# Six lines moved in the order lists of an attention and expert kernel on one Trainium2 core

## The reference, cut to what matters

```python
B, H, S, D = 2, 8, 576, 64
scores = D ** -0.5 * q @ k.T                  # per batch and head, 576 x 576
kth = the 32nd largest score of each row
scores = where(scores >= kth, scores, -1e9)   # top 32 of 576
attn = exp(scores - max); attn /= attn.sum() + 1e-9
x = (attn @ v) as 1152 x 512
x = silu(x @ w_in) @ w_out                    # 512 -> 2048 -> 512
P = exp(x @ w_gate - max), then 8 rounds of row and column normalisation
out = sum over 8 experts of P[:, e] * (relu(x @ w1[e]) @ w2[e])   # 512 -> 1024 -> 512
```

## Time and profile before

| | |
|---|---|
| median of three runs | 1304.44 us |
| profiled execution | 1304.42 us, its span 1302.6 |
| TensorE busy | 1265.2 us (97%) |
| VectorE busy | 653.2 us (50%) |
| ScalarE busy | 458.6 us (35%) |
| GpSimd busy | 365.7 us (28%) |
| chain that ended last | TensorE 79%, VectorE 16% |

### The profile page before, as it was taken

How to read it: one execution, slowest core, us unless ns; L and a number is a source line. 1 busy time by engine, 2 the same in 40 slices (tenths; PEclk the granted TensorE clock), 3 DMA queues, 4 the chain that set the end, 5 groups by cost and what they waited for, 6 DMA issues and landing times.

```text
span 1302.6 us, 21366 instructions
## 1 busy us (share of the span) xinstructions
PE 1265.2 (97%) x8109; PEld 1119.5 (86%) x8109; DVE 653.2 (50%) x1557; ACT 458.6 (35%) x960; POOL 365.7 (28%) x319
## 2 busy tenths in 40 slices
PE   6999999999999999999999999999999999999999
PEld 5777787887887998899899899898898898998997
DVE  5999999999998237322222222222222222222222
ACT  4776666766766233022022032031131130220210
POOL 2774434524434223033032031131131130230300
PEclk9999999999999999999999999999999999999999
DMA  4875664654544643021021120020120220210001
GB/s 129 275 245 181 255 221 127 231 186 171 208 178 156 259 162 98 1 65 50 17 65 33 32 64 32 32 64 17 48 64 1 64 64 0 64 60 5 0 0 72
DMA packets 72929, 130.14 MB, mean 100 GB/s; under 512 B 42016, under 2 KB 42016, under 8 KB 63648
## 3 DMA queue, kind: packets, MB, share of 16 engines
q1 hardware_dynamic: 72864, 129.27, 29.3%
HBM read 110.12 MB, written 19.14 MB: 99 GB/s over the span
## 4 chain that ended last, share of the span: by engine, by line
PE 79%; DVE 16%; ACT 1%; SPq 1%; DMA 1%; issue 1%; POOL 1%; ACTq 0%; DVEq 0%
PE banks L409 25%; PE banks L411 24%; PE banks L410 24%; DVE stats L862 7%; DVE rest L873 6%; PE banks L477 2%; PE banks L444 1%; PE banks L453 1%; DVE g_f L927 1%; PE banks L470 1%; DMA q_nat<-in_q_dram 1%; SPq L333 1%; PE banks L500 0%; ACT pT L705 0%; PE banks L425 0%
## 5 line engine op out<-in xcount | busy, mean ns | idle before, releaser
L822 ACT ACTIVATE h_hi<-banks 128x384 fp32r<-128x384 f32 x192 | 94.4, 492 | 624.7 <-PE banks L411 624.7
L409 PE MATMUL banks<-x_lo,wu_hi 128*128 128x384 f32 x768 | 257.2, 335 | 0.0
L411 PE MATMUL banks<-x_hi,wu_hi 128*128 128x384 f32 x768 | 256.8, 334 | 0.0
L410 PE MATMUL banks<-x_hi,wu_lo 128*128 128x384 f32 x768 | 256.8, 334 | 0.0
L988 DVE SCALAR_TENSOR_TENSOR h_lo<-banks,h_hi 128x384 fp32r<-128x384 f32 x192 | 106.8, 557 | 281.7 <-ACT h_hi L822 281.7
L1087 POOL TENSOR_TENSOR wu_lo<-wu_raw,wu_hi 128x512 fp32r<-128x512 f32 x76 | 95.9, 1299 | 526.1 <-ACT wu_hi L761 519.1
L1030 DVE SCALAR_TENSOR_TENSOR y_acc<-banks,plan_e,y_acc 128x512 f32<-128x512 f32 x135 | 101.3, 751 | 272.3 <-PE banks L411 272.3
L409 PE MATMUL banks<-wd_lo,h_hi 128*128 128x512 f32 x576 | 227.9, 396 | 0.0
L411 PE MATMUL banks<-wd_hi,h_hi 128*128 128x512 f32 x576 | 227.8, 396 | 0.0
L410 PE MATMUL banks<-wd_hi,h_lo 128*128 128x512 f32 x576 | 227.8, 396 | 0.0
L862 DVE MAX8 stats<-rest 128x8 f32<-128x576 f32 x216 | 156.1, 750 | 0.7
(11 more groups left out here) (103 smaller groups left out, 1804.7 us busy)
## 6 DMA issues: line engine op xcount, KB each, us to landing
wu_raw<-in_moe_w_dram SPq DMA_DIRECT2D x32, 512.0 KB, 3.7
wd_raw<-in_moe_w_dram SPq DMA_DIRECT2D x32, 512.0 KB, 3.7
wu_hi<-kept_up_hi SPq DMA_DIRECT2D x14, 1024.0 KB, 5.6
wu_lo<-kept_up_lo SPq DMA_DIRECT2D x14, 1024.0 KB, 8.0
wd_hi<-kept_down_hi SPq DMA_DIRECT2D x14, 1024.0 KB, 6.3
wd_lo<-kept_down_lo SPq DMA_DIRECT2D x14, 1024.0 KB, 8.4
q_nat<-in_q_dram SPq DMA_DIRECT2D x64, 72.0 KB, 2.3
wu_raw<-in_moe_w_in_dram SPq DMA_DIRECT2D x8, 512.0 KB, 5.3
```

Of the source, the lines that this page charges most:

```text
L409: pe.matmul(to, a_hi, b_lo, start=first, stop=False)
L410: pe.matmul(to, a_lo, b_hi, start=False, stop=False)
L411: return pe.matmul(to, a_hi, b_hi, start=False, stop=last)
L822: act.activation(h_hi[:, f, CH * c:CH * (c + 1)], ps_up[:, at % UBANKS, 0:CH], ACT.Relu).then_inc(h_hi_done, 1)
```

## The change

It moves lines in the lists of all five queues and touches no instruction itself.

- SP: the load of the first half of the next unit goes out at the step behind the one that begins a unit (it was two behind), the second half and the keeping two behind (three). Half 0 of the last "down" unit of the first expert thereby falls into the loop, half 1 stays behind it.
- TensorE: the weighing of tile s-3 stands ahead of the scores of tile s+1.
- ScalarE: `copy_scores(s+1)` stands behind `exp_scores(s-2)`, a high part of g and `copy_output(s-3)`.
- GpSimd: the low pieces stand behind the low parts of the outputs and of g, and they are those of ScalarE's same step, not of the step before.

```diff
 # SP
+                if split_at(step - 1):
+                    stream, n = split_at(step - 1)
+                    load_split(stream, n + 1, 0)
                 if split_at(step - 2):
                     stream, n = split_at(step - 2)
-                    load_split(stream, n + 1, 0)
-                if split_at(step - 3):
-                    stream, n = split_at(step - 3)
                     load_split(stream, n + 1, 1)
                     if n < SLOTS:
                         keep_unit(stream, n)
...
-            for half in range(2):
-                load_split("down", UQ + 1, half)
+            load_split("down", UQ + 1, 1)
 # TensorE
+                if 0 <= step - 3 < ALL:
+                    weigh_values(step - 3)
                 if step + 1 < ALL:
                     scores_of(step + 1)
-                if 0 <= step - 3 < ALL:
-                    weigh_values(step - 3)
 # ScalarE
                 take_slice(slice_at(step, 0))
-                if step + 1 < ALL:
-                    copy_scores(step + 1)
                 if 0 <= step - 2 < ALL:
                     exp_scores(step - 2)
                 g_high(slice_at(step - 1, 1))
                 if 0 <= step - 3 < ALL:
                     copy_output(step - 3)
+                if step + 1 < ALL:
+                    copy_scores(step + 1)
                 split_pieces(pieces_at(step, 0))
 # GpSimd
                     lower_scores(step - 2)
-                if step <= ALL:
-                    split_pieces(pieces_at(step - 1, 0))
-                    split_pieces(pieces_at(step - 1, 1))
                 if step % NT == 3 and NT <= step < ALL + NT:
                     output_lows(step // NT - 1, 2)
                 g_low(slice_at(step - 1, 0))
                 g_low(slice_at(step - 1, 1))
+                if step < ALL:
+                    split_pieces(pieces_at(step, 0))
+                    split_pieces(pieces_at(step, 1))
```

## The result

The changed kernel took 1319.2 us (median of 5 runs, 1318.45 to 1321.45), the kernel before 1306.11 on the same chip (5 runs, 1304.42 to 1306.95). The ratio is 1.0107, 95% interval 1.0093 to 1.012: slower, as forecast, with the forecast time of 1318.8 us met to 0.4 us. The profiled execution of the changed kernel took 1318.84 us, its span is 1317.0; before it was 1302.6, so that 14.4 us are to be found in the trace.

What follows compares the result with a forecast made beforehand. VectorE's searches, later with TensorE, were taken to set the attention stage's pace, TensorE alone the expert stage's. 1304.4 + 11.0 (GpSimd's low pieces) + 3.4 (TensorE's order) + 0 gave 1318.8 us, range 1307 to 1323.

Steps and rivals of the forecast that it cites:

- The ring: GpSimd and ScalarE wait in turn, steps 2 to 16: rounds of 6.00 us against VectorE's 5.28, 11.0 us lost.
- Its high bound: Upper bound of the ring's cost, with more time for output copies and a later copy_scores in seven steps: 13.7 us.
- VectorE's wait in the ring: VectorE would wait for copy_scores (L862) or an exponential (L888), some 0.8 us a step from about step 5 on.
- TensorE's order: Weighing first makes TensorE wait for ScalarE's copy: 0.68 us in five rest-tile steps without a first slice, 3.4 us.
- The five others without a slice: There TensorE later waits 1.06 us for VectorE's slice, which takes up the 0.68 us: cost 0.
- ScalarE's order: Exponential ahead of copy_scores on ScalarE: could return the 0.3 us wait at L888, taken as 0.
- SP's order: Earlier weight loads could mend only one late head, VectorE's 0.7 us wait at 84 us; nothing if VectorE waits anyway.
- The sum: Whole kernel: 1304.4 + 11.0 + 3.4 + 0 = 1318.8 us, 1.1% slower, chance 0.58.
- the one without a ring (1307.8): Rival: GpSimd isn't held up, only TensorE's part is left, 1307.8 us (+0.26%), chance 0.12.
- the ring alone (1315.4): Rival: GpSimd's low pieces cost VectorE time as forecast, TensorE's part is hidden, 1315.4 us, chance 0.14.

Runs made afterwards that it cites:

- e8: The kernel before with SP's edit alone: 1303.37 us, ratio 0.9979.
- e11: The kernel before with SP's and ScalarE's edits: 1303.42 us, ratio 0.9981.
- e10: The kernel before with SP's and ScalarE's edits, and the weighing ahead of the scores only in steps with a first slice: 1303.68 us, ratio 0.9986.
- e2: The changed kernel with only GpSimd's edit undone: 1309.51 us, ratio 1.0025.
- e5: The kernel before with TensorE's edit alone (weighing ahead of the scores): 1319.88 us, ratio 1.0096.
- e3: The changed kernel with ScalarE's first high piece of a step made ahead of the exponential, up to step 72: 1311.79 us, ratio 1.0037.
- e4: The changed kernel, but GpSimd makes the second low piece of ScalarE's step before and the first of the same step: 1310.14 us, ratio 1.003.
- e9: The kernel before with TensorE's and ScalarE's edits: 1313.07 us, ratio 1.0053.
- e12: The kernel before with ScalarE's edit alone: 1305.93 us, ratio 0.9997.
- e6: The kernel before with the weighing ahead of the scores only in steps with a first slice: 1310.85 us, ratio 1.0036.
- e7: The changed kernel with TensorE's edit undone: 1314.97 us, ratio 1.0064.
- e1: The kernel before with GpSimd's edit alone: 1316.35 us, ratio 1.0079.

## Why the prediction was right, point by point

The whole change can be walked in steps of one edit each, by medians: before 1306.3, SP's edit 1303.4 (e8), ScalarE's too 1303.4 (e11), the weighing ahead where a slice covers it 1303.7 (e10), the weighing ahead everywhere 1309.5 (e2), GpSimd's edit 1319.2 (the changed kernel). That is 2.9 less, nothing, 0.3, 5.8 and 9.7 more, 12.9 together, where the first comparison measured 13.1; the runs are from several chips. In this order SP's and ScalarE's edits stand ahead of TensorE's; in another order the shares differ, as e5 shows.

- **The ring** was right in place, kind and length: rounds of 5.89 and 6.08 for 6.00 and 6.16. It cost 9.32 us by tile 18, where 11.0 were forecast. Fifteen rounds took 89.7 for 91.1 us, as three links were 0.02 to 0.06 shorter than the rows they were taken from, and the whole began 0.5 us earlier. Its high bound adds up to 13.8, not 13.7.
- **VectorE's wait in the ring** was named wrongly. The prediction had copy_scores (L862) or L888. In the seven steps that have one it is the copy of the output; the scores are short in five, by 0.3 us at most.
- **TensorE's order** was right in its place and in its unit: five rest tiles, 0.68 forecast, 0.67 to 0.70 measured in four of them. The term was mis-sized at 3.4 us; it measured 5.0, because in one of the five the clock fell behind the gap and the loss was 1.5 us larger (2.22 less 0.69). In e2, e3, e4 and e9 it fell behind another of the five, and the loss there is 2.2 or 2.3 us, about 0.7 at the four others. The sum had no term for the clock. The five others without a slice cost nothing, as forecast.
- **ScalarE's order** at 0 was right as an edit by itself (e12). Beside TensorE's edit it is worth 6.8 us (e5 and e9), since without it that edit holds back the copy of the output; the changed kernel without it was not tried. The prediction costed each edit against the kernel before and did not ask what an edit prevents beside another.
- **SP's order** at 0 was wrong by itself: 2.9 us by medians (e8). The prediction bounded the gain with the 0.7 us of one profile in which the clock was granted in full. That holds nearly for such executions (1.1 us); what it left out is that the clock can fall behind the wait for the head (e6, e9, e12), which costs some 1.5 us more. In the changed kernel that wait is gone too, as forecast. How much of the gain the ring leaves there was not tried; by their places the gain lies inside the steps that the ring slows.
- **The sum** came out at 1318.8 for 1319.2 partly since errors cancelled: 1.7 too much for the ring, 1.6 too little for TensorE. That the two cancelled was luck. It was also made against an execution of 1304.42 us with the clock granted in full, while the kernel before has its median at 1306.1 here and 1306.0 to 1306.3 later; by profiles the change costs 14.4 us, by medians 13.1.
- Of the rivals, the one without a ring (1307.8) has its like in e2, 1309.5, and the ring alone (1315.4) in e7, 1315.0. Both were well placed, but neither was this change.

## What to carry to other kernels

Where one engine's queue takes a piece made by another in the same step, write down the links of the ring and compare the sum with the pace of the engine that sets the time: at 5.98 us against 5.28 it cost 9.3 us in some sixteen steps, at 5.4 it cost 1.9. An order on one engine is a contract with the others, so cost an edit also beside its partners: the instruction that is made earlier helps only where its copy stands early on the next engine. Put work that needs no copy between a transpose and the product that needs it, and before a gain is bounded by a wait in one profile, look whether the clock fell behind that wait in other executions.

## What the runs showed of the hardware

A gap of 0.78 us on TensorE was followed by a fall of its clock, though not each time. The gap, ahead of the weighing of a rest tile, stands five times between 120 and 400 us in the changed kernel, the work around it being much the same, and the clock fell behind one of them. It fell once in e2, e3, e4 and e9 and twice in e5, which have these gaps too, each time for some 4 us that begin within 4 us behind such a gap. In the eight profiles without these gaps (before, e1, e6, e7, e8, e10, e11 and e12) every stretch of 2 us from 120 to 400 has a clock of 1.00. All 14 profiles have the same gap once more at a rest tile between 422 and 439 us; there it fell in e3, e5, e7, e8 and e9. That is 12 falls behind 44 such gaps. The same kernels have gaps of 0.6 to 1.7 us elsewhere from 120 to 400 us, in the changed kernel four of 0.78 us ahead of an ordinary weighing (from 200.44 to 359.52) among them, and no fall stands behind those, so that the length alone does not decide.

Ahead of 120 us the clock fell behind longer waits: for q at 81 us in e6, e9 and e12 (2.06 to 2.72 us), but not in before (2.07); and in the five kernels with a new order on GpSimd (the changed one, e1, e3, e4 and e7), in the changed one from 26 to 30 us, behind a wait of 3.41 us for the exponential. That fall did not lengthen the ring, whose round there took 5.91 us. Where the loss behind a fall can be told apart (the fall between 120 and 400 us in the changed kernel, e2, e3, e4 and e9, and the one at 82 us in e9), it was about 1.5 us.

The Trainium skill (TensorE: Matmul & The Clock Gate, section A second HAM failure mode: psum-queue depth-cycling) tells of a kernel whose TensorE often pauses briefly between groups of products and whose clock goes to and fro between its levels. The trace agrees in that a pause of 0.78 us can be followed by a fall; in the changed kernel it was one of five, and which of them it strikes stays open.
